# Softmax division moved behind the value product: a factor spread by DMA, one multiply of x on GpSimd, and shorter lags

## The chip, the cores and the metric

One core of a Trainium2 chip runs the whole program. The metric is the device time in microseconds (us) of one launch; lower is better. The engines are called PE (TensorE), PEld (its weight load), DVE (VectorE), ACT (ScalarE), POOL or Pool (GpSimd) and SP (the queue that issues the DMAs).

## What is computed

Attention over 16 heads of 768 tokens and 64 features, in which a query sees only the keys with the same 6-bit hash of sign bits, followed by two MLPs of 512, 2048 and 512 features over 1536 tokens:

```python
q_bits = (np.einsum('bhsd,dk->bhsk', q, proj) > 0)      # the same for k; a bucket is the 6 bits
mask = q_bucket[:, :, :, None] == k_bucket[:, :, None, :]
scores = np.where(mask, scale * np.matmul(q, k.transpose(0, 1, 3, 2)), -1000000000.0)
attn = np.exp(scores - np.max(scores, axis=-1, keepdims=True))
attn = attn / (np.sum(attn, axis=-1, keepdims=True) + 1e-09)
x = np.matmul(attn, v)                                  # heads side by side: (1536, 512)
x = gate_1(x @ w_in) @ w_out                            # gate_1: 0, (h + 1)^2 / 4 or h
return (lambda h: h - np.tanh(h))(x @ w_in2) @ w_out2
```

## The kernel before

All products are done in pairs of a rounded high part and a remainder ("hi" and "lo"), so nearly every operand is split by a rounding copy and a subtraction. The kernel has two stages. This case is about the first, the attention; the MLPs follow from about 260 us on and are PE's products one after the other.

**Pairs and steps.** The 16 heads are worked off as 8 pairs. A pair has 12 tiles of 128 queries by 768 keys (`PT_TILES`), tiles 0 to 5 of its first head (s = 0) and 6 to 11 of its second (s = 1). Each engine runs its own loop over n = 0 to 11 in `pair(p)`; I call one turn a step. In step n PE makes the scores of tile n (`scores`, 4 matmuls), then one third of a value product of an older tile (`weighted_values`, 4 matmuls), then the 6 transposes of another older tile (`transposes`). After steps 5 and 7 it also makes the bit products of the next pair (`bit_products`). Which older tile it is, is set by lags: the operation for tile o stands in step o + lag, and runs over into the next pair.

**A tile's way.** DVE takes the masked scores from PSUM and finds the row's least value (`clamp`), ACT takes the exponential and the row's sum (`exponent`), DVE inverts the sums of three tiles at a time (`invert`, a `tensor_scalar` called row_den here and a reciprocal), Pool multiplies the tile by the inverse (`normalise`, lag 3), PE transposes it (lag 5) into two PSUM banks e = 0 and 1, ACT rounds each bank (`parts_hi`), DVE subtracts (`parts_lo`), and only then is that bank free for the next tile's transposes. After three tiles PE has what it needs for the value product (lag 9, over three steps); ACT copies its lower half out (`lower_half`) and DVE adds it to the upper one (`fold`, lag 11) into x_pair. x_pair holds both heads: partitions 0 to 63 the first, 64 to 127 the second, with the queries along the free side. In step 9 ACT rounds the last pair's x_pair (`round_x`), and Pool subtracts (`split_x`).

**Pool and SP.** The order of every engine is written out by hand in `pair`. Between its `normalise` instructions Pool splits q, k and v of the coming heads (`split_q`, `split_k`, `split_v`): in steps 0 and 1 for the second head of this pair, in steps 6 and 7 for the first head of the next. ACT makes the rounded k for it (`round_k`). SP waits for the split, copies the rounded q and the bits into place (`copy_q_hi`, `copy_bits`) and then issues the next loads; PE's first scores of a head wait for those copies. The last pair is followed by a drain: the loops run once more for what lags, PE mixes in the first products of the MLP (`early_hidden`), and Pool splits the MLP's weights (`split_w`), the first two of them already in steps 5 and 7 of the last pair.

## Time and profile before

| | |
|---|---|
| three runs, median (range) | 784.14 us (783.81 to 784.57) |
| the profiled execution | 784.89 us, of it 783.0 us in the profile's span |
| PE busy, by the page | 757.5 us (97%) |
| DVE, ACT, POOL busy | 422.3 (54%), 356.3 (46%), 327.2 us (42%) |
| granted clock of PE | 0.995 over the span |

The shares are means over both stages. Up to about 245 us DVE, ACT and Pool are busy most of the time too; behind it PE alone is.

### The profile page before, as it was taken

To read this page: it belongs to the slowest core of one execution; us is meant where nothing else is said; L and a number is where in the kernel's file an instruction comes from. 1 tells how busy PE (TensorE), PEld (TensorE's weight loads), DVE (VectorE), ACT (ScalarE), POOL (GpSimd) and SP (SyncE) were. 2 spreads that over 40 slices of the span, in tenths; PEclk is the share of its full clock that TensorE was granted. 3 is DMA by queue.
4 is the path that set the end of the run, shared out by engine and by line. 5 is a ranking of instruction groups with operands and counts; after the bars stand their busy time and mean duration, and the time that the engine had idled before them with its cause. 6 is when DMAs were issued, how large, how long until landed. Compare 5 with 4: busy or idle time off the path is not lost.

```text
span 783.0 us, 11765 instructions
## 1 busy us (share of the span) xinstructions
PE 757.5 (97%) x3712; PEld 636.5 (81%) x3712; DVE 422.3 (54%) x757; ACT 356.3 (46%) x701; POOL 327.2 (42%) x267
## 2 busy tenths in 40 slices
PE   4999999999999999999999999999999999999998
PEld 2788888888888888878887888878888888888886
DVE  2899999999997565353334455551123221231213
ACT  2889889889887333343334333331122221221212
POOL 4789889889899995000000176770000000000000
PEclk8999999999999999999999999999999999999999
DMA  5533523523222333000000032220000000010001
GB/s 191 173 118 106 162 76 106 162 76 106 82 83 75 128 120 109 0 1 1 0 1 0 0 107 85 102 81 1 0 1 32 23 0 0 0 54 0 0 0 54
DMA packets 17864, 47.25 MB, mean 60 GB/s; under 512 B 2288, under 2 KB 4464, under 8 KB 17840
## 3 DMA queue, kind: packets, MB, share of 16 engines
q1 hardware_dynamic: 17840, 46.94, 18.7%
q8 instruction: 14, 0.23, 0.1%
q14 instruction: 10, 0.08, 0.0%
HBM read 38.87 MB, written 3.15 MB: 54 GB/s over the span
## 4 chain that ended last, share of the span: by engine, by line
PE 81%; POOL 5%; issue 5%; DVE 4%; ACT 3%; DMA 2%; SPq 1%; DVEq 0%; POOLq 0%; ACTq 0%
PE ps L498 33%; PE ps L575 30%; PE ps L475 5%; PE ps L489 5%; PE ps L461 2%; PE ps L464 2%; PE ps L432 2%; POOL probs L355 2%; POOL k_b L340 1%; ACT probs L620 1%; DMA k_raw<-kk 1%; DVE g_raw L814 1%; DVE row_den L744 1%; ACT g_hi L702 1%; POOL q_b L312 1%
## 5 line engine op out<-in xcount | busy, mean ns | idle before, releaser
L498 PE MATMUL ps<-x_hi,w 128*128 (+1 forms) x768 | 249.7, 390 | 0.0
L822 DVE TENSOR_TENSOR g_lo<-g_raw,g_hi 128x512 fp32r<-128x512 f32 x96 | 72.6, 756 | 261.5 <-ACT g_hi L702 261.5
L702 ACT ACTIVATE g_hi<-g_raw 128x512 fp32r<-128x512 f32 x96 | 60.7, 632 | 287.9 <-PE ps L575 262.7
L498 PEld LDWEIGHTS ps<-x_hi,w 128*128 128x128 f32 x768 | 144.1, 188 | 29.7
L498 PE MATMUL ps<-x_lo,w 128*128 (+1 forms) x384 | 149.4, 389 | 0.0
L575 PE MATMUL ps<-g_hi,w 128*128 128x512 f32 x384 | 125.2, 390 | 2.5 <-DVE g_lo L822 2.5
L575 PE MATMUL ps<-w,g_hi 128*128 128x512 f32 x384 | 118.2, 389 | 0.0
L312 POOL TENSOR_SCALAR w<-stage 128x1024 fp32r<-128x1024 f32 x32 | 39.0, 1217 | 159.1 <-PE ps L575 157.9
L752 DVE TENSOR_TENSOR p_lo<-ps,p_hi 128x384 fp32r<-128x384 f32 x192 | 97.9, 552 | 9.7 <-ACT p_hi L630 8.1
L355 POOL TENSOR_SCALAR probs<-probs,row_inv 128x768 f32<-128x768 f32 x96 | 86.9, 909 | 23.9 <-DVE row_inv L746 22.9
L630 ACT ACTIVATE p_hi<-ps 128x384 fp32r<-128x384 f32 x192 | 84.7, 489 | 25.0 <-PE ps L475 22.9
L736 DVE TENSOR_SCALAR_CACHE_REDUCE clamped<-ps 128x768 f32<-128x768 f32 x96 | 91.0, 949 | 6.0 <-PE ps L464 5.9
L620 ACT ACTIVATE probs<-clamped,row_min 128x768 f32<-128x768 f32 x96 | 90.2, 939 | 8.6 <-DVE clamped L736 8.6
L475 PE MATMUL ps<-ident,probs 128*128 128x128 f32 x576 | 82.3, 277 | 7.4 <-POOL probs L355 3.8
L575 PEld LDWEIGHTS ps<-g_hi,w 128*128 128x128 f32 x384 | 72.1, 188 | 19.1 <-DVE g_lo L822 4.1
L370 POOL TENSOR_TENSOR w<-stage,w 128x1024 fp32r<-128x1024 f32 x32 | 83.8, 2620 | 2.7
L575 PEld LDWEIGHTS ps<-w,g_hi 128*128 128x128 f32 x384 | 72.1, 188 | 14.9
L498 PEld LDWEIGHTS ps<-x_lo,w 128*128 128x128 f32 x384 | 72.1, 188 | 14.7
L475 PEld LDWEIGHTS ps<-ident,probs 128*128 128x128 f32 x576 | 65.6, 140 | 20.8 <-DVE p_lo L752 11.0
L575 PE MATMUL ps<-g_lo,w 128*128 128x512 f32 x192 | 74.7, 389 | 0.0
L575 PE MATMUL ps<-w,g_lo 128*128 128x512 f32 x192 | 74.7, 389 | 0.0
L814 DVE TENSOR_TENSOR g_raw<-g_mid,g_raw 128x512 f32<-128x512 f32 x48 | 52.3, 1089 | 33.5 <-ACT g_mid L696 33.5
(48 smaller groups left out, 902.6 us busy)
## 6 DMA issues: line engine op xcount, KB each, us to landing
stage<-weights SPq DMA_DIRECT2D x32, 512.0 KB, 3.3
qk_raw<-qk SPq DMA_DIRECT2D x16, 384.0 KB, 3.5
q_raw<-qq SPq DMA_DIRECT2D x16, 384.0 KB, 3.1
k_raw<-kk SPq DMA_DIRECT2D x16, 384.0 KB, 3.8
q_a<-q_b SPq DMA_DIRECT2D x16, 192.0 KB
v_raw<-v SPq DMA_DIRECT2D x16, 192.0 KB, 2.7
out<-stage SPq DMA_DIRECT2D x12, 256.0 KB, 2.1
q_b<-bits SPq DMA_DIRECT2D x16, 54.0 KB
```

What stands on the lines that cost most here:

```text
L355: pool.tensor_scalar(probs[:, o % QT, :], probs[:, o % QT, :], row_inv[:, o % QT:o % QT + 1], 1.0, ALU.mult, ALU.mult).then_inc(probs_read ...
L370: pool.tensor_tensor(w[:, slot, 1, :], stage[:, i, :], w[:, slot, 0, :].bitcast(F32), ALU.subtract).then_inc(w_ready, 1)
L475: last = nc.tensor.transpose(part_bank(o, e)[:, j * P:(j + 1) * P], probs[:, o % QT, kt * P:(kt + 1) * P], ident[:, :])
L498: last = nc.tensor.matmul(ps[:, f % H_BANKS, :], w[:, f, wp, k * P:(k + 1) * P], xs[:, k, bass.ds(t * TOK, TOK)], start=(k == 0 and wp == ...
L575: last = nc.tensor.matmul(ps[:, 4 + m, :], a, b, start=(f == 0 and i == 0), stop=(f == FC - 1 and i == 2))
L620: nc.scalar.activation(probs[:, n % QT, :], clamped[:, n % 2, :], ACT.Exp, bias=row_min[:, n % QT:n % QT + 1], scale=-1.0, accum_out=row_s ...
L630: nc.scalar.activation(p_hi[:, k % 2, HT * e:HT * (e + 1), i, :], part_bank(o, e).rearrange("p (j q) -> p j q", j=HT), ACT.Copy)\
L702: nc.scalar.activation(g_hi[:, slot, :], g_raw[:, slot, :], ACT.Copy).then_inc(g_hi_ready, 1)
L736: nc.vector.tensor_scalar(clamped[:, n % 2, :].rearrange("p (c n) -> p c n", c=2), score_bank(TURNS.index(n)), FLOOR, None, ALU.min, ALU.m ...
L752: nc.vector.tensor_tensor(p_lo[:, k % 2, HT * e:HT * (e + 1), i, :], part_bank(o, e).rearrange("p (j q) -> p j q", j=HT), p_hi[:, k % 2, H ...
L814: nc.vector.tensor_tensor(g_raw[:, slot, :], g_mid[:, slot, :], g_raw[:, slot, :], ALU.add)\
L822: nc.vector.tensor_tensor(g_lo[:, slot, :], g_raw[:, slot, :], g_hi[:, slot, :].bitcast(F32), ALU.subtract).then_inc(g_split, 1)
```

## The change

`normalise` is gone, and PE transposes the exponentials as they are, as soon as ACT has made them. The inverse of the row sums is made once for a head (6 tiles) instead of once for three tiles. SP stores it to memory (`store_inv`, 128 partitions of 6 numbers) and loads it back, so that every one of the head's 64 partitions of x_pair has all 768 factors beside its queries (`spread_inv`, into inv_wide). Pool then multiplies x_pair by it, in two halves of 384 queries (`scale_x`, steps 5 and 9 of the next pair), where the inverse is read with a step of 6 numbers. ACT's rounding and Pool's subtraction of x go in halves too. Pool makes the rounded k itself, which ACT did. The lags go from 5, 9 and 11 to 4, 8 and 10. ACT and DVE do the parts of a step ahead of the fold, and DVE inverts last. In the drain DVE scales the last pair's x.

```diff
@@ -54,10 +54,10 @@
-SCALE_LAG = 3
-TRANSPOSE_LAG = 5
-PV_LAG = 9
-FOLD_LAG = 11
+TRANSPOSE_LAG = 4
+PV_LAG = 8
+FOLD_LAG = 10
+SCALE_TURNS = [5, 9]
...
-            row_sum = sb("row_sum", [P, QT], F32, att)
-            row_den = sb("row_den", [P, QT], F32, att)
-            row_inv = sb("row_inv", [P, QT], F32, att)
+            row_sum = sb("row_sum", [P, 2, QT], F32, att)
+            row_den = sb("row_den", [P, 2, QT], F32, att)
+            row_inv = sb("row_inv", [P, 2, QT], F32, att)
+            inv_wide = sb("inv_wide", [P, S], F32, att)
+            x_tiles = x_pair[:, :].rearrange("p (o q) -> p o q", o=QT)
+            inv_tiles = inv_wide[:, :].rearrange("p (q o) -> p o q", o=QT)
...
+            def store_inv(p, s):
+
+                sp.wait_ge(inv_ready, 2 * p + s + 1)
+                sp.dma_start(factors[2 * p + s, :].rearrange("(q o) -> q o", o=QT), row_inv[:, s, :])\
+                    .then_inc(inv_stored[s], 16)
+
+            def spread_inv(p, s):
+
+                sp.wait_ge(inv_stored[s], 16 * (p + 1))
+                if s == 0:
+                    wait_from(sp, x_scaled, 2 * p)
+                sp.dma_start(inv_wide[s * D:(s + 1) * D, :], factors[bass.ds(2 * p + s, 1), :].broadcast_to([D, S]))\
+                    .then_inc(inv_spread, 16)
...
+                first = isinstance(p, int) and p == 0
                 sp.wait_ge(qk_split, 2 * p + 2)
                 copy_q_hi(1)
                 copy_bits(1)
+                if not first:
+                    store_inv(p - 1, 1)
+                if not last:
+                    load_qk(2 * p + 3, 1)
+                if not first:
+                    spread_inv(p - 1, 1)
                 if last:
                     return
-                load_qk(2 * p + 3, 1)
...
                 copy_q_hi(0)
                 copy_bits(0)
+                store_inv(p, 0)
                 if not before:
                     load_qk(2 * p + 4, 0)
+                spread_inv(p, 0)
                 sp.wait_ge(v_split, 2 * p + 2)
                 load_v(2 * p + 3, 1)
...
             load_w(0, 0)
             load_w(1, 1)
+            for s in range(2):
+                store_inv(PAIRS - 1, s)
+                spread_inv(PAIRS - 1, s)
...
             def split_k(p, s):
+                pool_round(k_a[:, s, :], k_raw[:, s, :]).then_inc(k_hi_ready, 1)
...
-            def normalise(p, o):
-
-                wait_alone(pool, inv_ready, 4 * p + o // HT + 1, pool_passed)
-                pool.tensor_scalar(probs[:, o % QT, :], probs[:, o % QT, :], row_inv[:, o % QT:o % QT + 1], 1.0,
-                                   ALU.mult, ALU.mult).then_inc(probs_ready, 1)
-
-            def split_x(p):
-                pool.wait_ge(x_hi_ready, p + 1)
-                pool.tensor_tensor(x_lo_flat[:, bass.ds(rows(p), S)], x_pair[:, :],
-                                   x_hi_flat[:, bass.ds(rows(p), S)].bitcast(F32), ALU.subtract)\
-                    .then_inc(x_ready, 1)
+            def scale_x(p, half):
+
+                cols = slice(half * HT, (half + 1) * HT)
+                wait_alone(pool, folded, 4 * p + 3 + half, pool_passed)
+                wait_alone(pool, inv_spread, 32 * (p + 1), pool_passed)
+                pool.tensor_tensor(x_tiles[:, cols, :], x_tiles[:, cols, :], inv_tiles[:, cols, :], ALU.mult)\
+                    .then_inc(x_scaled, 1)
+
+            def split_x(p, half):
+                pool.wait_ge(x_hi_ready, 2 * p + half + 1)
+                run = bass.ds(rows(p) + half * HALF, HALF)
+                pool.tensor_tensor(x_lo_flat[:, run], x_pair[:, half * HALF:(half + 1) * HALF],
+                                   x_hi_flat[:, run].bitcast(F32), ALU.subtract).then_inc(x_ready, 1)
...
-                    old = trailing(p, n, SCALE_LAG)
-                    if old and not (drain and n >= SCALE_LAG):
-                        normalise(*old)
+                    old = trailing(p, 0, 1)
                     if not drain:
+                        if old and n in SCALE_TURNS:
+                            scale_x(old[0], SCALE_TURNS.index(n))
...
+                        if old and n == 7:
+                            split_x(old[0], 0)
                         if n == 7 and not last:
                             split_k(p + 1, 0)
                         if n == 10 and not last:
                             scale_q(p + 1, 1)
+                        if old and n == 10:
+                            split_x(old[0], 1)
                         if n == 11:
                             split_v(p, 1)
-                        if last and n in (5, 7):
-                            split_w((n - 5) // 2)
-                    if n == 9 and not drain:
-                        old = trailing(p, 0, 1)
-                        if old:
-                            split_x(old[0])
+                        if last and n in (5, 8):
+                            split_w((n - 5) // 3)
...
             pair(PAIRS - 1)
-            pair(PAIRS, drain=True)
...
             def transposes(p, o):
-                pe.wait_ge(probs_ready, PT_TILES * p + o + 1)
+                pe.wait_ge(exp_done, PT_TILES * p + o + 1)
...
-            def round_k(p, s, tiles_before):
+            def round_k(p, s):
                 act.wait_ge(qk_loaded[s], 32 * (p + 1))
-                wait_from(act, scores_ready, tiles_before)
                 nc.scalar.activation(k_a[:, s, :], k_raw[:, s, :], ACT.Copy).then_inc(k_hi_ready, 1)
-            def round_x(p):
-                act.wait_ge(folded, 4 * (p + 1))
-                nc.scalar.activation(x_hi_flat[:, bass.ds(rows(p), S)], x_pair[:, :], ACT.Copy)\
-                    .then_inc(x_hi_ready, 1)
+            def round_x(p, half):
+                act.wait_ge(x_scaled, 2 * p + half + 1)
+                nc.scalar.activation(x_hi_flat[:, bass.ds(rows(p) + half * HALF, HALF)],
+                                     x_pair[:, half * HALF:(half + 1) * HALF], ACT.Copy).then_inc(x_hi_ready, 1)
...
-                act.wait_ge(folded, 4 * PAIRS - 1 + half)
+                act.wait_ge(x_last_scaled, half + 1)
...
-                    if n == 9 and not drain:
-                        old = trailing(p, 0, 1)
-                        if old:
-                            round_x(old[0])
-                    if n in (6, 9) and drain:
-                        round_last_x((n - 6) // HT)
-                    old = trailing(p, n, FOLD_LAG)
-                    if n % HT == HT - 1 and old and not (drain and n >= FOLD_LAG):
-                        lower_half(old[0], old[1] // HT)
                     old = trailing(p, n, TRANSPOSE_LAG)
                     if old and not (drain and n >= TRANSPOSE_LAG):
                         parts_hi(*old)
+                    old = trailing(p, n, FOLD_LAG)
+                    if old and old[1] % HT == 0 and not (drain and n >= FOLD_LAG):
+                        lower_half(old[0], old[1] // HT)
+                    old = trailing(p, 0, 1)
+                    if old and n - 1 in SCALE_TURNS and not drain:
+                        round_x(old[0], SCALE_TURNS.index(n - 1))
+                    if drain and n in (FOLD_LAG - 5, FOLD_LAG - 2):
+                        round_last_x((n - FOLD_LAG + 5) // HT)
                     if not drain:
-                        if n == 0:
-                            round_k(p, 1, PT_TILES * p)
-                        if n == 6 and not (isinstance(p, int) and p == PAIRS - 1):
-                            round_k(p + 1, 0, PT_TILES * p + QT)
                         exponent(p, n)
...
-            def invert(p, k):
-
-                cols = slice((k % 2) * HT, (k % 2 + 1) * HT)
-                dve.wait_ge(exp_done, PT_TILES * p + HT * (k + 1))
-                nc.vector.tensor_scalar(row_den[:, cols], row_sum[:, cols], 1e-9, None, ALU.add).then_inc(den_ready, 1)
-                dve.wait_ge(den_ready, 4 * p + k + 1)
-                nc.vector.reciprocal(row_inv[:, cols], row_den[:, cols]).then_inc(inv_ready, 1)
+            def invert(p, s):
+
+                dve.wait_ge(exp_done, PT_TILES * p + QT * (s + 1))
+                nc.vector.tensor_scalar(row_den[:, s, :], row_sum[:, s, :], 1e-9, None, ALU.add).then_inc(den_ready, 1)
+                dve.wait_ge(den_ready, 2 * p + s + 1)
+                wait_from(dve, inv_stored[s], 16 * p)
+                nc.vector.reciprocal(row_inv[:, s, :], row_den[:, s, :]).then_inc(inv_ready, 1)
...
-                if k == 0:
-                    wait_from(dve, x_ready, p)
+                if k < 2:
+                    wait_from(dve, x_ready, 2 * p - 1 + k)
                 nc.vector.tensor_tensor(x_pair[r:r + D, c:c + HALF], ps[0:D, PV0 + k % 2, 0:HALF], low[:, k % 2, :], ALU.add)\
                     .then_inc(folded, 1)
+            def scale_last_x(half):
+
+                cols = slice(half * HT, (half + 1) * HT)
+                dve.wait_ge(folded, 4 * PAIRS - 1 + half)
+                dve.wait_ge(inv_spread, 32 * PAIRS)
+                nc.vector.tensor_tensor(x_tiles[:, cols, :], x_tiles[:, cols, :], inv_tiles[:, cols, :], ALU.mult)\
+                    .then_inc(x_last_scaled, 1)
...
-                    if n in (6, 9) and drain:
-                        split_last_x((n - 6) // HT)
                     if not drain:
                         clamp(p, n)
-                    old = trailing(p, n, FOLD_LAG)
-                    if n % HT == HT - 1 and old and not (drain and n >= FOLD_LAG):
-                        fold(old[0], old[1] // HT)
-                    old = trailing(p, n, HT)
-                    if n % HT == 0 and old and not (drain and n >= HT):
-                        invert(old[0], old[1] // HT)
                     old = trailing(p, n, TRANSPOSE_LAG)
                     if old and not (drain and n >= TRANSPOSE_LAG):
                         parts_lo(*old)
+                    old = trailing(p, n, FOLD_LAG)
+                    if old and old[1] % HT == 0 and not (drain and n >= FOLD_LAG):
+                        fold(old[0], old[1] // HT)
+                    if drain and n in (FOLD_LAG - 6, FOLD_LAG - 3):
+                        scale_last_x((n - FOLD_LAG + 6) // HT)
+                    if drain and n in (FOLD_LAG - 5, FOLD_LAG - 2):
+                        split_last_x((n - FOLD_LAG + 5) // HT)
+                    old = trailing(p, n, QT)
+                    if n % QT == 0 and old and not (drain and n > 0):
+                        invert(old[0], old[1] // QT)
                     if not drain and n in BITS_AFTER and not last:
                         threshold(p + 1, BITS_AFTER.index(n))
```

On Pool, in the middle pairs (pairs 1 to 6), steps 6 to 9. Before:

```order
L77 ISA [waits scores_ready]
L312 TENSOR_SCALAR q_b<-q_raw 128x768 [waits q_scaled]
L327 TENSOR_TENSOR q_a<-q_raw,q_b 128x768 [waits q_hi_ready]
L355 TENSOR_SCALAR probs<-probs,row_inv 128x768 [waits inv_ready]
L340 TENSOR_TENSOR k_b<-k_raw,k_a 128x768 [waits k_hi_ready]
L355 TENSOR_SCALAR probs<-probs,row_inv 128x768 [waits inv_ready]
L77 REGISTER_ALU
L355 TENSOR_SCALAR probs<-probs,row_inv 128x768 [waits inv_ready]
L360 ISA [waits x_hi_ready]
L360 TENSOR_TENSOR x_lo<-x_pair,x_hi 128x768
```

And with the change, from step 5 on (L390 is `scale_x`, L396 `split_x`, L344 the rounding copy):

```order
L390 TENSOR_TENSOR x_pair<-x_pair,inv_wide 128x384 [waits inv_spread]
L77 REGISTER_ALU
L77 ISA [waits scores_ready]
L344 TENSOR_SCALAR q_b<-q_raw 128x768 [waits q_scaled]
L359 TENSOR_TENSOR q_a<-q_raw,q_b 128x768 [waits q_hi_ready]
L394 ISA
L396 ISA [waits x_hi_ready]
L396 TENSOR_TENSOR x_lo<-x_pair,x_hi 128x384
L344 TENSOR_SCALAR k_a<-k_raw 128x768
L373 TENSOR_TENSOR k_b<-k_raw,k_a 128x768 [waits k_hi_ready]
```

The three `normalise` instructions left the stretch; the first half of x is now multiplied ahead of the split of the next head, and its remainder is made inside it, between q and k.

On SP, at the top of a middle pair. Before:

```order
L238 DMA q_a<-q_b 64x768 [waits qk_split]
L244 DMA q_b<-bits 18x768
L244 DMA k_b<-bits 18x768
L227 ISA
L227 DMA q_raw<-qq 128x768
L227 DMA k_raw<-kk 128x768
L271 REGISTER_ALU
L230 ISA [waits v_split]
L230 DMA v_raw<-v 128x384
```

And with the change:

```order
L244 DMA q_a<-q_b 64x768 [waits qk_split]
L250 DMA q_b<-bits 18x768
L250 DMA k_b<-bits 18x768
L255 ISA
L256 ISA [waits inv_ready]
L256 DMA factors<-row_inv 128x6
L233 ISA
L233 DMA q_raw<-qq 128x768
L233 DMA k_raw<-kk 128x768
L261 REGISTER_ALU
L264 DMA inv_wide<-factors 64x768 [waits inv_stored1]
```

The store of the last head's inverse stands behind the three copies, the loads behind it, and the spread behind the store's landing.

## Rows read from the trace of the kernel before

**Rows 1.** Busy time by stretch: pair 0, pairs 1 to 6 (five periods), the rest.

```profile
core 0: us, PE busy (x) PEld busy (x) DVE busy (x) ACT busy (x) POOL busy (x), PEclk, DMA share, GB/s
16.50:39.80 23.30, 21.60 (x111) 17.71 (x111) 19.03 (x45) 16.89 (x37) 17.33 (x18) 0.89 0.64 185
52.80:198.90 146.10, 142.21 (x882) 126.42 (x881) 139.61 (x311) 127.21 (x276) 129.99 (x126) 1.00 0.37 115
199.00:243.80 44.80, 42.10 (x265) 37.80 (x263) 43.00 (x97) 38.86 (x86) 40.90 (x38) 1.00 0.27 85
```

**Rows 2.** Timeline of PE: the bit products behind step 5 of pairs 1 and 6.

```profile
52.77 0.49 PE L432 MATMUL ps<-qk_raw,mask_s 128*72 128x384 f32 x1
...
198.93 0.81 PE L432 MATMUL ps<-qk_raw,mask_s 128*72 128x384 f32 x2
```

**Rows 3.** The chain that ended last, pair 5: start us, us, what.

```profile
169.86 1.29 PE ps L432 x4
171.15 0.35 PE ps L461 x2
171.50 0.36 PE ps L464 x2
171.86 0.70 PE ps L489 x4
172.57 0.66 PE ps L475 x6
```

**Rows 4.** Who waited for whom, 52.8 to 198.9 us: total, times, longest.

```profile
PEld ps L475 <- DVE p_lo L752: 9.8, 25, 0.7
...
PE ps L475 <- POOL probs L355: 2.1, 5, 0.4
```

**Rows 5.** Timeline of DVE in pair 5: start, duration, instruction.

```profile
158.17 0.99 DVE L744 TENSOR_SCALAR row_den<-row_sum 128x3 f32<-128x3 f32 x1
...
162.05 0.95 DVE L736 TENSOR_SCALAR_CACHE_REDUCE clamped<-ps 128x768 f32<-128x768 f32 x1
...
162.93 0.55 DVE L763 TENSOR_TENSOR x_pair<-ps,low 64x384 f32<-64x384 f32 x1
163.43 1.02 DVE L752 TENSOR_TENSOR p_lo<-ps,p_hi 128x384 fp32r<-128x384 f32 x2
164.37 0.95 DVE L736 TENSOR_SCALAR_CACHE_REDUCE clamped<-ps 128x768 f32<-128x768 f32 x1
...
165.24 0.69 DVE L744 TENSOR_SCALAR row_den<-row_sum 128x3 f32<-128x3 f32 x1
...
172.93 0.16 DVE L744 TENSOR_SCALAR row_den<-row_sum 128x3 f32<-128x3 f32 x1
```

**Rows 6.** Timeline of POOL in the same pair.

```profile
158.12 1.01 POOL L349 TENSOR_TENSOR v_s<-v_raw,v_s 128x384 fp32r<-128x384 f32 x1
...
160.45 0.83 POOL L312 TENSOR_SCALAR q_b<-q_raw 128x768 fp32r<-128x768 f32 x1
...
164.07 1.84 POOL L340 TENSOR_TENSOR k_b<-k_raw,k_a 128x768 fp32r<-128x768 f32 x1
```

**Rows 7.** Timeline of ACT in the same pair.

```profile
163.67 0.94 ACT L620 ACTIVATE probs<-clamped,row_min 128x768 f32<-128x768 f32 x1
...
165.57 0.94 ACT L620 ACTIVATE probs<-clamped,row_min 128x768 f32<-128x768 f32 x1
```

**Rows 8.** DMA issues of the whole run: KB each, median us to landing.

```profile
k_raw<-kk SPq DMA_DIRECT2D x16, 384.0 KB, 3.8
...
v_raw<-v SPq DMA_DIRECT2D x16, 192.0 KB, 2.7
out<-stage SPq DMA_DIRECT2D x12, 256.0 KB, 2.1
```

**Rows 9.** Timeline of SP's queue in the same pair.

```profile
165.94 0.53 SPq L238 DMA_DIRECT2D q_a<-q_b  x1
...
167.32 0.70 SPq L244 DMA_DIRECT2D k_b<-bits  x1
```

**Rows 10.** Costliest groups of the whole run: busy, mean ns.

```profile
L370 POOL TENSOR_TENSOR w<-stage,w 128x1024 fp32r<-128x1024 f32 x32 | 83.8, 2620 | 2.7
```

21 lines of the change are left out of this document (13 added, 8 removed).

## The prediction

> **What bounds the kernel now.** I read the busy times by stretch first [rows 1]: from 52.8 to 198.9 us PE is busy 97% of the time and DVE 96%, so neither has room, and the attention is where the two wait for each other. The two bit products that bound this stretch stand at the same place of pairs 1 and 6 [rows 2], so it holds five pairs, and a pair takes (198.93 - 52.77) / 5 = 29.2 us.
>
> Next, what would a pair take if PE never waited? The chain, where it runs along PE [rows 3], gives a step: scores 0.35 + 0.36, a third of a value product 0.70, transposes 0.66, together 2.07 us; and 1.29 us for a bit product, of which a pair has two. 12 x 2.07 + 2 x 1.29 = 27.4 us. So a pair has 1.8 us of stalls. The waits say whose they are [rows 4]: the weight loads of the transposes wait 9.8 us in five pairs, 2.0 a pair, for DVE's p_lo, which frees their PSUM bank, and the transposes 2.1 us, 0.4 a pair, for Pool's `normalise` (these overlap a little). The larger part is thus a late DVE, not a late Pool.
>
> Why is DVE late? Its own step [rows 5]: clamp to the next instruction 162.93 - 162.05 = 0.88, two p_lo 164.37 - 163.43 = 0.94, together 1.82 us in a step of 2.07. There is 0.25 us of room a step. A fold takes 163.43 - 162.93 = 0.50 of it. And row_den, an instruction on 3 numbers a partition, takes 0.16 us once, but 0.99 and 0.69 us at other times. The longer two end at 159.16 and 165.93; Pool's instructions that were running [rows 6] end at 158.12 + 1.01 = 159.13 and 164.07 + 1.84 = 165.91. So row_den waits until Pool's instruction in progress is over. That is 0.8 and 0.5 us lost on the path from p_lo to the transposes.
>
> **What the change does to a pair.** Pool loses 12 `normalise` a pair, and with them the wait of 0.4 us a pair on PE disappears. The path from the exponential to the transposes has nothing but ACT in it now. That is sure.
>
> DVE: 4 row_den and 4 reciprocals become 2 and 2. But they stand in steps 0 and 6, just where Pool runs four instructions on end for a head: q_b 0.83, q_a and k_b 1.84 [rows 6], and the rounded k as long as q_b. A row_den that falls there at random waits on average (0.83^2 + 1.84^2) / (2 x 2.67) = 0.76 us, at least 0, at most 1.84. In sum 2 x 0.76 against some 1.3 for the two of before: DVE gains only what two short pairs of instructions cost, under 0.7 us a pair. The place matters too: behind p_lo, the delay meets the next clamp and the next p_lo. As p_lo may come about 0.6 us late before PE feels it (2.07 - 1.82 and the slack between its end and the transposes, an estimate), a row_den that costs 0.16 + 0.2 for the reciprocal + 0.76 = 1.1 us stalls PE by 0.5 in step 0. In step 6 the same is hidden by the bit product behind step 7, 1.29 us of PE against one short DVE instruction. The folds of steps 1 and 4 add perhaps 0.1.
>
> ACT: exponential to exponential it takes 165.57 - 163.67 = 1.90 us [rows 7] of 2.07. The two rounded k of a pair leave it; x comes in two halves, of which the one in step 10 stands behind a `lower_half` and should cost PE about 0.1. So 1.8 us of stalls become 0.6 (0.5 + 0.1, the rest hidden); a pair takes 28.0 us. **Per pair: -1.2 us.**
>
> **The new round trip.** The half of step 5 needs the factor, which needs Pool, SP, two DMAs one behind the other. I count from PE's first scores of a pair, t = 0. Pool reaches the split at about t = 2.4: step 10 of the pair before starts at 10 x 2.07 + 2 x 1.29 = 23.3, its transposes 1.4 later, ACT's two parts, lower half and half of x end at about 27.0 (an estimate from one ACT step of 1.9), and Pool's remainder and v follow, 1.0 + 1.6, to 29.6, which is 2.2 to 2.4 of the next pair. It takes 5.5 us to 7.9. SP's copies take from 165.94 to 167.32 + 0.70 [rows 9], 2.1 us, to 10.0. The store lands like the smallest HBM store, 2.1 us [rows 8], at 12.1; the spread like v, of the same 192 KB, 2.7, at 14.9, with the loads of q and k ahead of it at most 1 us later. A DMA that writes 24 bytes a partition is not in the trace: its landing lies between nothing and the longest row, 3.8, and I take the store's. The multiply has the size of v's remainder, 1.0 us [rows 6]: done at 15.9. ACT wants it at about 16.5 (step 6, behind its parts). Then Pool goes on: q 2.75, the remainder of x 1.0, k 2.75 to 22.4, copies to 24.5, landed some 1.7 later (an estimate from the first head) at 26.3; PE wants it at 27.4. So the trip fits, with about 1 us to spare, and costs nothing while it does.
>
> The multiply reads inv_wide in steps of 24 bytes, which no row of before does. Below it is bounded by 0.5 (half of v's remainder), above by the 1.84 of an instruction of twice the size. I take 1.0, as its sizes are those of v's remainder. By the Trainium skill (GPSIMD Engine Reference, section Performance pitfalls for Q7 kernels), a read of SBUF by steps of over 8 bytes costs about half as much again on GpSimd; no trace here shows it. By that rule the multiply would take 1.5 instead of 1.0 us, and the sum would stay where it is, with half of the spare time gone.
>
> For the row_den the Trainium skill (SBUF — State Buffer, section Who interferes with whom) names an exclusive lock of the port pair that VectorE and GpSimd share, for `tensor_scalar` among others, held for a whole instruction. The trace agrees with it [rows 5, 6]. The rule goes further than the rows: it lets a VectorE instruction with both inputs in SBUF wait in the same way, which concerns the last pair's multiply only.
>
> **The ends.** Pair 0: a shorter lag puts one group of transposes and one third of a value product, 1.36 us [rows 3], into the start, where PE has 23.3 - 21.6 = 1.7 us idle [rows 1], and takes it from the drain, where PE is full. I take -0.8, between 0 and -1.7. The stretch from 199.0 to 243.8 is 44.8 / 28 = 1.6 pairs: -1.9. In the last pair Pool splits two weights of 2.62 us [rows 10] and a rounding each between the two multiplies; its second multiply is then ready about 1 to 2 us after ACT asks for it in step 10, with no bit products in that pair to hide it: +1.0. In the drain SP loads the third weight only behind the last spread, and DVE has one more multiply, of 1 us and a possible 2.6 of Pool's instruction, ahead of the first gate of the MLP: +0.4, between 0 and +3. The MLPs themselves are untouched.
>
> **Sum:** 5 x -1.2 = -6.0, -1.9, -0.8, +1.0, +0.4 = -7.3 us. The profiled execution took 784.89, 0.75 above the median of the three runs. 784.9 - 7.3 = 777.6, and 0.75 less on the scale of the median: 776.8.
>
> **Rivals.**
> 1. *Forecast*, stalls fall to 0.4 to 1.0 a pair: 773 to 781, chance 0.47.
> 2. *All stalls go.* If row_den finds Pool between instructions, or PE feels none of it: 27.4 a pair, -1.8 x 6.6 = -11.9, -0.8 in the start: 772 with the ends' losses, 769 without them and with 1.7 gained in the start. For it speaks that PE then waits for nothing that the change left; against it, that DVE would still be busy some 27 of 27.4 us. Chance 0.18.
> 3. *The gain is eaten* by row_dens at their upper bound: 2 x 1.84 puts DVE at 29 us a pair, the same as now. With the ends' +1.4 and -0.8, 781 to 785, chance 0.15.
> 4. *Slower: a late factor.* Where: Pool's multiply of step 5, with q, k and the copies of the next head queued behind it and ACT's exponentials behind the rounding of step 6. The spare time is about 1 us and the stalls of before 1.8, so from 2.9 us of lateness on it decides against the change. Both DMAs at 3.8 instead of 2.1 + 2.7 are +2.8, the multiply at 1.84 +0.8: 3.6 late, a pair of 27.4 + 2.6 = 30.0, +0.8 x 6.6 = +5.3, and with the ends about 790. A middle value of these is 785 to 788. Chance 0.16.
> 5. *The slow stride alone*: the multiply lies between v's remainder, 1.0, and the 1.84 of twice the size [rows 6], so about 0.5 us more for each half, and with the loads ahead of the spread ACT gets x 0.5 to 0.9 us late in step 6. Stall up to 0.5 a pair, 6.6 x 0.5 = 3.3: 780. Chance 0.04, beside what 1 holds of it. The GPSIMD Engine Reference of the Trainium skill, cited above, is what speaks for it.
>
> **Numbers.** The likeliest is 776.8. Its own range is 773 to 781; the range for 8 in 10 takes in rivals 2 and 3 and the start of 4: 769 to 787. A measurement of this kernel tells about 0.2%, 1.6 us, from no change. Faster by more than that (below 782.6): 1, 2, 5 and half of 3, 0.76. Within it: the rest of 3 and a little of 4, 0.09. Slower: 0.15.
>
> **What would show it.** In the profile after: a pair of about 28.0 us between bit products; no wait of the transposes for Pool, and that for DVE's p_lo down from 2.0 to about 0.7 a pair; two row_dens a pair of 0.2 to 2 us, each ending with an instruction of Pool; the multiply at about 1.0 us and ACT's rounding of x without a wait for it, except once in the last pair. Wrong would be: PE's scores waiting for the copied bits (rival 4), ACT waiting for x in every pair, or the multiply at 1.5 and more. The step I trust least is the round trip's spare microsecond.

## The result and the profile after

The changed kernel took 793.18 us (median of 4 runs, 790.28 to 794.71), the kernel before 783.97 us beside it (783.63 to 784.57): a ratio of 1.0108, 95% interval 1.0093 to 1.0123. It is slower by 9 us, where 776.8 had been forecast and 787 was the end of the range. The profiled execution took 794.71 us, the slowest of the four, with a span of 792.5 us, 9.5 more than before.

Busy time by stretch, after the change; the stretches are those of [rows 1], shifted to the same places of the program, with one for the drain:

```profile
core 0: us, PE busy (x) PEld busy (x) DVE busy (x) ACT busy (x) POOL busy (x), PEclk, DMA share, GB/s
16.50:39.80 23.30, 21.51 (x109) 18.15 (x110) 19.13 (x38) 15.37 (x34) 13.13 (x13) 0.85 0.66 187
55.30:202.60 147.30, 143.25 (x883) 126.31 (x882) 138.93 (x291) 123.56 (x272) 97.69 (x90) 1.00 0.45 123
202.60:248.70 46.10, 41.80 (x266) 38.06 (x263) 42.84 (x89) 38.11 (x86) 30.41 (x27) 1.00 0.24 70
```

Five pairs took 147.3 us instead of 146.2. Pool was rid of a quarter of its work there, 130.0 to 97.7 us. DVE was rid of 0.7 us in five pairs and no more. The timeline of PE has the bit products that answer to [rows 2]:

```profile
55.28 1.13 PE L466 MATMUL ps<-qk_raw,mask_s 128*72 128x384 f32 x3
...
202.56 1.13 PE L466 MATMUL ps<-qk_raw,mask_s 128*72 128x384 f32 x3
```

From such marks the whole run can be cut up: the bit products of pair 0, those of pairs 1 and 6, PE's first product of the MLP with x (hidden), its first product of g (project), the end. The same cuts serve for every kernel below. The differences are of the marks themselves, before rounding.

| us | before | after | difference | predicted |
|---|---|---|---|---|
| start to the bits of pair 0 | 25.2 | 26.2 | +1.0 | 0 |
| bits of pair 0 to bits of pair 1 | 27.5 | 29.1 | +1.5 | -0.8 |
| a pair, mean of five | 29.23 | 29.46 | +0.23 (x5: +1.1) | -1.2 (x5: -6.0) |
| bits of pair 6 to first hidden | 47.4 | 49.1 | +1.7 | -0.9 |
| first hidden to first project | 20.8 | 25.0 | +4.2 | +0.4 |
| first project to the end | 515.8 | 515.8 | 0 | 0 |

The first row is the start's own scatter (24.1 to 28.2 us over all kernels here, with no order by their edits). It goes largely with the clock that PE was granted from 5 to 28 us: 0.85 in the kernel before and 0.78 after, 0.85 in experiment 9, which has the shortest start (24.1), and 0.70 in experiment 7 (27.8), though 12, the longest, had 0.78. The waits of the changed kernel from 55.3 to 202.5 us, which answer to [rows 4]:

```profile
PEld ps L509 <- DVE p_lo L780: 9.9, 30, 1.1
...
PE ps L509 <- DVE p_lo L780: 4.0, 5, 0.8
...
ACT x_hi L679 <- POOL x_pair L390: 2.2, 4, 0.7
```

No transpose waits for Pool any more: that step came true. But PE waits as long for p_lo as before, at fewer and longer stops. One is in the timelines of DVE, POOL and PE of a pair:

```profile
162.70 1.32 DVE L771 TENSOR_SCALAR row_den<-row_sum 128x6 f32<-128x6 f32 x1
164.15 0.19 DVE L774 RECIPROCAL row_inv<-row_den 128x6 f32<-128x6 f32 x1
164.35 0.96 DVE L764 TENSOR_SCALAR_CACHE_REDUCE clamped<-ps 128x768 f32<-128x768 f32 x1
...
165.24 1.02 DVE L780 TENSOR_TENSOR p_lo<-ps,p_hi 128x384 fp32r<-128x384 f32 x2
```

```profile
162.16 1.84 POOL L359 TENSOR_TENSOR q_a<-q_raw,q_b 128x768 fp32r<-128x768 f32 x1
```

```profile
165.84 1.01 PE L509 MATMUL ps<-ident,probs 128*128 128x128 f32 x6 [0.80 <-DVE p_lo L780]
```

row_den ends at 164.02, with Pool's q_a at 164.00; six numbers a partition took 1.32 us. Clamp and p_lo follow late, and PE stops for 0.80 us. The ten row_dens of the stretch took 0.95 us in the mean; the twenty of before, on half as many numbers, 0.50. Half the instructions, each twice as long: DVE won nothing. The mean hides a fixed pattern: the row_den of step 0 took 1.32 or 1.33 us in each of the five pairs, always to the end of q_a, and the one of step 6 took 0.17 to 0.78.

The round trip, in the timelines of SP's queue, POOL and ACT in pair 5 (PE's first scores of the pair at 158.97):

```profile
166.74 0.53 SPq L244 DMA_DIRECT2D q_a<-q_b  x1
167.31 0.79 SPq L250 DMA_DIRECT2D q_b<-bits  x1
168.15 0.73 SPq L250 DMA_DIRECT2D k_b<-bits  x1
169.19 0.37 SPq L256 DMA_DIRECT2D factors<-row_inv  x1
169.76 0.35 SPq L233 DMA_DIRECT2D q_raw<-qq  x1
170.20 0.38 SPq L233 DMA_DIRECT2D k_raw<-kk  x1
171.84 0.56 SPq L264 DMA_DIRECT2D inv_wide<-factors  x1
```

```profile
176.35 1.21 POOL L390 TENSOR_TENSOR x_pair<-x_pair,inv_wide 128x384 f32<-128x384 f32 x1 [7.25 <-DMA inv_wide<-factors]
```

```profile
177.69 0.53 ACT L679 ACTIVATE x_hi<-x_pair 128x384 f32 x1 [0.53 <-POOL x_pair L390]
```

The inverse was ready at 164.34 and its store was issued at 169.19: 4.9 us it stood behind SP's wait for the split. Then store 2.65 us (169.19 to 171.84, where the spread leaves), spread 4.5 (to the multiply's start at 176.35), multiply 1.21. How the first two share the time differs from pair to pair: at the same place of the pair before, the store landed in 1.4 us and the spread in 5.4, here in 2.6 and 4.3. Their sum does not: from the store's issue to the spread's landing it took 6.9 to 7.1 us at this place in each of the five pairs. The page's table of DMA issues has the medians of the whole run; its first row answers to that of [rows 8]:

```profile
k_raw<-kk SPq DMA_DIRECT2D x16, 384.0 KB, 5.2
...
inv_wide<-factors SPq DMA_DIRECT2D x16, 192.0 KB, 4.6
...
factors<-row_inv SPq DMA_DIRECT2D x16, 3.0 KB, 1.7
```

So the store is a short transfer as a rule, and the spread, behind the 768 KB of q and k, the long one.

The last pair has the longest stop. Pool splits a weight there, DVE's row_den waits for it, and PE's scores wait for the clamp behind (timelines of POOL, DVE, PE):

```profile
235.49 2.38 POOL L405 TENSOR_TENSOR w<-stage,w 128x1024 fp32r<-128x1024 f32 x1
```

```profile
236.17 1.72 DVE L771 TENSOR_SCALAR row_den<-row_sum 128x6 f32<-128x6 f32 x1
```

```profile
239.05 0.61 PE L495 MATMUL ps<-k_a,q_a 128*128 128x384 f32 x2 [2.00 <-DVE clamped L764]
```

In the drain SP issued the third and fourth weight only behind the last spread, at 253.87, where the kernel before had issued them at 233.74 and 239.41. Pool got its weight at 258.73, and PE stopped twice (timelines of SP's queue, POOL, PE; then busy time by stretch):

```profile
253.04 0.47 SPq L264 DMA_DIRECT2D inv_wide<-factors  x1
253.87 0.90 SPq L320 DMA_DIRECT2D stage<-weights  x2
```

```profile
258.73 1.67 POOL L344 TENSOR_SCALAR w<-stage 128x1024 fp32r<-128x1024 f32 x1 [9.06 <-DMA stage<-weights]
```

```profile
267.42 0.50 PE L532 MATMUL ps<-x_hi,w 128*128 128x512 f32 x1 [1.25 <-POOL w L405]
...
272.23 0.50 PE L532 MATMUL ps<-x_hi,w 128*128 128x512 f32 x1 [1.78 <-POOL w L405]
```

```profile
272.20:276.70 4.50, 4.47 (x13) 3.55 (x14) 3.04 (x4) 1.75 (x3) 4.42 (x3) 0.62 0.31 117
272.70:276.00 3.30, 3.30 (x10) 2.56 (x9) 1.83 (x4) 1.75 (x3) 3.22 (x2) 0.50 0.42 159
```

Behind the second stop PE ran at half its clock from 272.7 to 276.0 us. At full clock it starts three of these products every 0.69 us, there every 1.28, so this alone is some 1.5 us of the drain's 4.2 (an estimate from the rows at the end of this document), and it belongs to this execution: no other kernel below had such a fall between hidden and project, and of the eleven others that issue the third weight as late, none needed more than 22.3 us there.

### The profile page after: what moved, and what is told of

The parts are those of the page before. It is cut to its first block, busy times and chain, and to the rows that moved or that the text cites. A ratio compares the mean times of both kernels' runs of the same rounds, so it can differ in the third digit from the quotient of the medians.

```text
span 792.5 us, 11668 instructions
## 1 busy us (share of the span) xinstructions
PE 760.3 (96%) x3712; PEld 638.3 (81%) x3712; DVE 428.5 (54%) x727; ACT 350.5 (44%) x693; POOL 273.4 (34%) x207
## 2 busy tenths in 40 slices
DMA packets 21447, 50.44 MB, mean 64 GB/s; under 512 B 4848, under 2 KB 7024, under 8 KB 21424
## 4 chain that ended last, share of the span: by engine, by line
PE 84%; DVE 5%; issue 3%; ACT 3%; DMA 2%; POOL 1%; SPq 0%; DVEq 0%; ACTq 0%; POOLq 0%
PE ps L532 32%; PE ps L609 30%; PE ps L509 7%; PE ps L523 6%; PE ps L495 4%; PE ps L498 4%; PE ps L466 2%; DVE p_lo L780 1%; DMA stage<-weights 1%; DVE row_den L771 1%; DVE clamped L764 1%; DMA k_raw<-kk 1%; DVE g_raw L852 1%; ACT g_hi L730 1%; POOL w L405 1%
## 5 line engine op out<-in xcount | busy, mean ns | idle before, releaser
L780 DVE TENSOR_TENSOR p_lo<-ps,p_hi 128x384 fp32r<-128x384 f32 x192 | 97.7, 550 | 12.9 <-ACT p_hi L664 12.7
L344 POOL TENSOR_SCALAR w<-stage 128x1024 fp32r<-128x1024 f32 x32 | 39.9, 1246 | 166.9 <-PE ps L609 155.1
L664 ACT ACTIVATE p_hi<-ps 128x384 fp32r<-128x384 f32 x192 | 84.8, 488 | 28.2 <-PE ps L509 27.3
L609 PEld LDWEIGHTS ps<-w,g_hi 128*128 128x128 f32 x384 | 72.1, 188 | 14.9
L852 DVE TENSOR_TENSOR g_raw<-g_mid,g_raw 128x512 f32<-128x512 f32 x48 | 54.2, 1129 | 33.5 <-ACT g_mid L724 33.5
L495 PE MATMUL ps<-k_a,q_a 128*128 128x384 f32 x192 | 60.5, 397 | 10.1 <-DMA k_b<-bits 6.2
```

Source lines behind the costliest of these rows:

```text
L495: nc.tensor.matmul(score_bank(turn)[:, c, :], q_a[:, s, q], k_a[:, s, c * HALF:(c + 1) * HALF], start=True, stop=False)
L609: last = nc.tensor.matmul(ps[:, 4 + m, :], a, b, start=(f == 0 and i == 0), stop=(f == FC - 1 and i == 2))
L664: nc.scalar.activation(p_hi[:, k % 2, HT * e:HT * (e + 1), i, :], part_bank(o, e).rearrange("p (j q) -> p j q", j=HT), ACT.Copy)\
L780: nc.vector.tensor_tensor(p_lo[:, k % 2, HT * e:HT * (e + 1), i, :], part_bank(o, e).rearrange("p (j q) -> p j q", j=HT), p_hi[:, k % 2, H ...
L852: nc.vector.tensor_tensor(g_raw[:, slot, :], g_mid[:, slot, :], g_raw[:, slot, :], ALU.add)\
```

## The experiments

Times are medians; the ratio is to the kernel before, run on the same chip in the same jobs (783.97 to 784.86 us), with its 95% interval. The cuts are those of the table above, each from one profiled execution. Two kernels with the same code in a cut tell how far one execution can be trusted there: pair 0 took 29.1 us in the changed kernel and 27.9 in 2, which differs from it only behind the last pair, but the mean of five pairs 29.46 and 29.42.

| kernel | us | ratio | pair 0 | a pair | pair 6 to hidden | hidden to project |
|---|---|---|---|---|---|---|
| before | 783.97 | | 27.5 | 29.23 | 47.4 | 20.8 |
| after | 793.18 | 1.0108 [1.0093, 1.0123] | 29.1 | 29.46 | 49.1 | 25.0 |
| 1 no row_den | 786.01 | 1.0013 [1.0004, 1.0023] | 26.7 | 29.22 | 48.0 | 21.4 |
| 2 weights first | 790.25 | 1.0072 [1.0055, 1.0088] | 27.9 | 29.42 | 50.2 | 20.4 |
| 3 both of these | 785.44 | 1.0017 [1.0002, 1.0032] | 26.7 | 29.16 | 47.4 | 20.3 |
| 4 before, no row_den | 780.11 | 0.9939 [0.9923, 0.9956] | 27.3 | 28.60 | 46.7 | 20.8 |
| 5 lags 5, 9, 11 | 783.47 | 0.9987 [0.9978, 0.9997] | 27.2 | 28.90 | 46.9 | 21.3 |
| 6 store first | 787.46 | 1.0040 [1.0020, 1.0059] | 28.4 | 29.22 | 47.7 | 21.8 |
| 7 store first, no row_den | 779.35 | 0.9926 [0.9910, 0.9943] | 26.7 | 28.02 | 46.2 | 22.2 |
| 8 all three edits | 777.42 | 0.9904 [0.9887, 0.9920] | 26.7 | 28.02 | 46.2 | 20.8 |
| 9 all three, lags 5, 9, 11 | 776.53 | 0.9902 [0.9885, 0.9919] | 26.6 | 28.14 | 46.0 | 20.8 |
| 10 no row_den, lags 5, 9, 11 | 778.50 | 0.9915 [0.9898, 0.9931] | 26.2 | 28.28 | 46.0 | 21.3 |
| 11 lags 4, 9, 11 | 835.85 | 1.0646 [1.0615, 1.0677] | 31.4 | 35.95 | 59.9 | 22.3 |
| 12 before, lags 4, 8, 10 | 805.45 | 1.0264 [1.0246, 1.0281] | 31.1 | 31.70 | 50.7 | 19.4 |
| 13 lags 4, 8, 11 | 785.36 | 1.0012 [1.0000, 1.0025] | 27.7 | 28.94 | 46.9 | 22.1 |
| 14 lags 5, 8, 10 | 803.45 | 1.0237 [1.0220, 1.0254] | 30.4 | 31.51 | 49.9 | 21.7 |
| 15 x_hi in step 11 | 799.99 | 1.0193 [1.0176, 1.0210] | 28.0 | 31.04 | 50.0 | 21.9 |
| 16 the same, lags 5, 9, 11 | 796.94 | 1.0150 [1.0127, 1.0173] | 27.7 | 30.71 | 51.5 | 21.4 |
| 17 x_hi in step 9 | 788.60 | 1.0056 [1.0040, 1.0073] | 28.2 | 29.30 | 47.4 | 21.4 |
| 18 all three, x_hi in step 9 | 775.26 | 0.9890 [0.9872, 0.9908] | 26.7 | 27.76 | 45.4 | 20.4 |

From the first project on every one of them took 515.8 to 516.0 us: the MLPs are untouched.

**1. Without row_den.** The sum of exponentials holds one exponential of 1, so 1e-9 vanishes in it.

```diff
-                nc.vector.tensor_scalar(row_den[:, s, :], row_sum[:, s, :], 1e-9, None, ALU.add).then_inc(den_ready, 1)
-                dve.wait_ge(den_ready, 2 * p + s + 1)
...
-                nc.vector.reciprocal(row_inv[:, s, :], row_den[:, s, :]).then_inc(inv_ready, 1)
+                nc.vector.reciprocal(row_inv[:, s, :], row_sum[:, s, :]).then_inc(inv_ready, 1)
```

> The changed kernel without row_den: the sum of a row is at least 1, so the added 1e-9 falls away in fp32, and the reciprocal reads the sums themselves. Everything else as in the changed kernel. Theory A (row_den, which waits for Pool's instruction in progress, is what keeps a pair at 29.5 us): the 0.95 us that it takes on average twice a pair go, a pair falls to 27.8 us or less, the total by 8 pairs x 1.6 to about 780. Rival B (the new order of ACT and DVE and the shorter lags keep the pair long): a pair stays above 29 us, the total within 2 us of the changed kernel, about 791.

7.2 us came back, between theory A and rival B. By the cuts it was 2.4 in pair 0, 1.1 from pair 6 to the MLP, 3.6 in the drain (of which some 1.5 are the clock of the one profiled execution, as above), but only 0.24 a pair. The stall had moved. In the timeline of ACT the exponentials now stand behind x_hi:

```profile
175.04 0.52 ACT L679 ACTIVATE x_hi<-x_pair 128x384 f32 x1 [1.63 <-POOL x_pair L390]
```

and the waits of five pairs have grown where those for p_lo shrank:

```profile
ACT x_hi L679 <- POOL x_pair L390: 7.3, 4, 2.4
PEld ps L509 <- DVE p_lo L778: 4.5, 18, 1.0
```

**2 and 3. Third and fourth weight loaded ahead of the last stores and spreads; the same without row_den.**

```diff
             load_w(1, 1)
+            for i in range(2):
+                sp.wait_ge(w_ready, i + 1)
+                load_w(2 + i, i)
             for s in range(2):
                 store_inv(PAIRS - 1, s)
                 spread_inv(PAIRS - 1, s)
-            with sp.Fori(1, FC) as c2:
+            with sp.Fori(2, FC) as c2:
```

> The changed kernel, with the loads of the third and fourth weight issued on SP ahead of the last pair's stores and spreads of the factor, as they were before the change. Theory A (the drain loses its 4 us because those loads stand behind the factor's round trip): the wait of PE for Pool's weights goes, the first projection of the MLP moves from 276.7 to about 271, the total falls by 4 to 6 us to about 788. Rival B (the drain is late for the multiply of x on DVE ahead of the first gate): the total falls by less than 1.5 us.

> Both edits, no row_den and the weights' loads first. If the two losses are independent, the total is the changed kernel less the sum of both gains: 793 - 12 - 5 = about 776, faster than the kernel before. If one hides the other, it is above that by what it hides.

With the weights first, hidden to project is 20.4 us instead of 25.0, as before the change, and the two stops are gone; 1.1 us went back ahead of the MLP. In the times it gave 2.9 us, less than the 4 to 6 of theory A, and the runs of the two touch (789.62 to 790.37 against 790.28 to 794.71). In 3 the 776 of two independent losses was missed by 9 us: beside experiment 1 the edit gave nothing that the times can tell (786.01 and 785.44): without row_den the drain took only 21.4 us as it was.

**4. The kernel before without row_den.**

```diff
-                nc.vector.tensor_scalar(row_den[:, cols], row_sum[:, cols], 1e-9, None, ALU.add).then_inc(den_ready, 1)
-                dve.wait_ge(den_ready, 4 * p + k + 1)
```

> The kernel before, without row_den, all else as it was. Theory A (row_den costs both kernels): the long row_dens of 0.99 and 0.69 us in a pair go, and the inverse reaches Pool earlier, so the total falls by about 1 us a pair, to about 776. Rival B (Pool's multiply of the tiles keeps PE waiting anyway): less than 2 us.

780.11 us, 0.63 a pair less, where theory A had 776. So row_den cost the kernel before about 4 us and the changed one 7: doing it half as often in longer pieces did not make it cheaper.

**5. The old lags in the changed kernel.** `TRANSPOSE_LAG`, `PV_LAG`, `FOLD_LAG` at 5, 9, 11.

> The changed kernel with the lags of before, 5, 9 and 11, all else as changed. Theory A (the shorter lags cost nothing in a pair and only move 1.4 us of PE's work from the drain to the start): a pair stays at 29.5 us, the start is up to 1.4 us shorter, the drain as much longer, the total within 1.5 us of the changed kernel, 791.7 to 794.7. Rival B (the shorter lags make the stalls): a pair falls below 29 us and the total by 3 us or more.

9.7 us came back, the rival's side by far, and against the prediction, in which the shorter lags were a gain.

**6, 7 and 8. The store ahead of the wait for the split.** 6 alone, 7 without row_den, 8 with the weights first as well.

```diff
+                if not first:
+                    store_inv(p - 1, 1)
                 sp.wait_ge(qk_split, 2 * p + 2)
                 copy_q_hi(1)
                 copy_bits(1)
                 if not first:
-                    store_inv(p - 1, 1)
-                if not last:
-                    load_qk(2 * p + 3, 1)
-                if not first:
                     spread_inv(p - 1, 1)
+                if not last:
+                    load_qk(2 * p + 3, 1)
```

> The changed kernel with SP's order at the top of a pair turned: the store of the factor first, ahead of the wait for the split, and the spread ahead of the loads of q and k. row_den stays. Theory A (with row_den in place the round trip just fits, as ACT waits only 0.5 us for x in step 6): Pool's multiply of step 5 comes 3 to 4 us earlier, PE gains less than 0.3 us a pair, the total is 791 to 793. Rival B (the trip already holds the pair up): the total falls by 4 us or more.

> The same order on SP, and no row_den. Theory A (without row_den the late factor is what keeps a pair at 29.2 us: ACT waited up to 2.4 us for x in step 6): that wait goes, a pair falls to 27.8 us, the total to about 786 - 8 x 1.3 = 776. Rival B (something else, such as p_lo waiting for p_hi, holds it): a pair stays above 28.8 us, the total above 783.

> All three edits: no row_den, the store first, the weights' loads first. If the theory of three losses holds (row_den, the late factor, the late weights), a pair takes 27.8 us, the first projection of the MLP comes at about 259 us instead of 276.7, and the total is 773 to 776, below the kernel before and below the kernel before without row_den (780.1).

6 alone gave 5.7 us, rival B's side in the total (4 or more) and theory A's in a pair (less than 0.3): the rest stood outside the five pairs. 7 and 8 missed their 776 and 773 to 776 by 3.4 and 1.4 us.

This is the reading of the pairs. Without row_den alone a pair takes 29.22 us, with the store first alone 29.22, with both 28.02. Each of the two costs hides the other: taken one at a time they are worth 0.24 us a pair, together 1.44. In 8 the timelines of SP's queue and POOL show the trip with the store made early and the spread ahead of the loads:

```profile
155.45 0.36 SPq L256 DMA_DIRECT2D factors<-row_inv  x1
...
161.44 0.56 SPq L264 DMA_DIRECT2D inv_wide<-factors  x1
162.21 0.41 SPq L233 DMA_DIRECT2D q_raw<-qq  x1
```

```profile
164.77 1.20 POOL L393 TENSOR_TENSOR x_pair<-x_pair,inv_wide 128x384 f32<-128x384 f32 x1 [3.30 <-DMA inv_wide<-factors]
```

The multiply starts 3.3 us after the spread's issue, not 4.5, with nothing ahead of it, and there is no wait of ACT for x left in five pairs. The edit did two things, the store ahead of the wait and the spread ahead of the loads; they were not run apart.

**9 and 10. The old lags with all three edits, and with row_den dropped alone.**

> The changed kernel without row_den, with the store of a head's inverse ahead of the wait for the split, with the third and fourth weight loaded before the last round trip, and with lags of 5, 9 and 11. Theory A (the lags cost time only through where VectorE's row_den meets Pool's long instructions): without row_den the lags are worth nothing in a pair, the period stays at 28.0 us, and only the half tile more of lag in the last pair and the drain moves the time, by up to 1 us either way: 776.5 to 778.5 us. Rival B (the longer lag gives ScalarE and VectorE room in each pair whatever row_den does): the period falls by the 0.5 us that the lags gave with row_den in place (29.46 to 28.9), the time by 3 us or more, to 774 us or less.

> The changed kernel without row_den and with lags of 5, 9 and 11, nothing else. Without row_den at 4, 8 and 10 it took 786.0 us, with row_den at 5, 9 and 11 it took 783.5. Theory A (both remove the same waits): the time lies within 1 us of the better one less the round trip's cost, 782 to 785 us. Rival B (two separate costs that add): 786.0 - 9.7, or some 776 to 778 us. In the waits ScalarE's wait for x on Pool, 7.3 us in all without row_den, tells how much of the rest is the round trip.

With all three edits the lags are worth less than a microsecond, and in a pair nothing (28.14 against 28.02), as theory A had it. But in 10 they gave 7.5 us without any row_den: theory A's ground, that they act through row_den, has fallen, and rival B came within 0.5 us of the time. That they act where the trip is tight is a reading that fits both, and the table of places below.

**11 and 12. Transposes alone at 4; the lags of 4, 8 and 10 in the kernel before.**

> The changed kernel with the transposes 4 tiles behind, and the products with v and the folds put back to 9 and 11. Theory A (what the old lags gave comes of the transposes' distance from the exponentials: with 5 the chain exp, transpose, rounding, p_lo has a tile more of slack against VectorE's row_den): little changes from the changed kernel, 791 to 794 us. Rival B (it comes of the fold and the products with v, which at 10 put the last fold of a head and the inverse closer to Pool's split and take a tile more from pair 0): most of the 9.7 us comes, 783 to 786 us.

> The kernel before with lags of 4, 8 and 10, and nothing else of the change. In it Pool still multiplies each tile of probabilities one turn ahead of the transpose (2.1 us of waits of the transposes for Pool in five pairs with a lag of 5). Theory A (the shorter lag by itself costs: a chain of one tile less): 787 to 793 us, with TensorE's waits for p_lo and for the scaled tiles grown by 3 us or more. Rival B (the short lag costs only together with the changed order of ScalarE and VectorE and the long row_den of the changed kernel): within 2 us of the kernel before, 783 to 786 us.

Both lie outside what either theory gave, for reasons of their own, which the waits name (over a stretch of some 147 us, which holds four pairs of 11 and not quite five of 12). In 11 a group's products with v end one step behind the transposes that want its buffer:

```profile
ACT p_hi L664 <- PE ps L523: 38.6, 16, 4.0
```

In 12 Pool's `normalise` has one step instead of two ahead of the transposes:

```profile
POOL probs L355 <- DVE row_inv L746: 26.1, 19, 2.9
...
PE ps L475 <- POOL probs L355: 10.9, 21, 1.3
```

So it is the change that makes the short lags possible, and 11 can't be read as a test of the fold.

**13 and 14. One lag put back at a time: the fold's to 11; the transposes' to 5.**

> The changed kernel with only the fold (and ScalarE's copy low ahead of it) put back from 10 tiles to 11; transposes stay at 4, products with v at 8. The old lags together gave 9.7 us (793.2 to 783.5). Theory A (it is where the fold falls: at 10 the copy low, 0.49 us, stands in step 10 of ScalarE beside x_hi, 0.51 us, and the fold, 0.55 us, stands in the step right behind VectorE's row_den; at 11 neither meets): most of it comes, 783 to 786 us. Rival B (it is the transposes' lag, the slack between exponential and transpose): it stays at 791 to 794 us.

> The changed kernel with only the transposes put back from 4 tiles to 5; products with v stay at 8, folds at 10. Theory A (the place of the fold): 791 to 794 us, no gain. Rival B (the slack between exponential and transpose, the chain p_hi, p_lo): 783 to 786 us. With the fold run beside it, the two tell whether the 9.7 us are one cause's or a sum.

The fold's lag alone brings 7.8 of the 9.7 us, 0.52 in a pair. 14 is lost to a wait that neither theory had: with transposes at 5 the products with v, at 8, come too soon for p_lo (15.2 us of waits in five pairs), so it says nothing of the rest.

**15 and 16. x_hi one step later, at lags 4, 8, 10 and at 5, 9, 11.** ACT's copy `low` and x_hi share step 10 at a fold lag of 10, and no step at 11; 15 parts them, 16 joins them.

```diff
-SCALE_TURNS = [5, 9]
+SCALE_TURNS = [5, 10]
...
-                        if old and n == 10:
+                        if old and n == 11:
                             split_x(old[0], 1)
```

> The changed kernel with the multiply of a head's second half in Pool's step 10 in place of 9, ScalarE's rounding x_hi in step 11 in place of 10, and Pool's x_lo in step 11; lags stay at 4, 8 and 10. ScalarE's step 10 then holds only one of low (0.49 us) and x_hi (0.51 us). Theory A1 (that meeting is what the lag of 10 costs): 5 of the 7 pairs' worth of some 0.5 us and the last pair come back, 788 to 791 us. Rival B (the meeting is harmless, as ScalarE has room): 792 to 794 us.

> The converse: lags of 5, 9 and 11 (783.5 us) with the same shift of the multiply to step 10 and of x_hi to step 11, where ScalarE's low of a fold at 11 stands. Theory A1 (low and x_hi in one step cost): 786 to 789 us. Rival B: 783 to 784.5 us.

Both got slower by much more than either theory said, 6.8 and 13.5 us. A little of it may be the clock: in the profiled executions of 14, 15 and 16 PE was once granted 0.50 for 3.3 us and more in the attention (in 15 at 187.8 to 191.1), in that of 11 three times. What 15 and 16 moved besides is Pool: it stands in its queue at x_lo until x_hi is done, with v and the next head's split behind it. The waits of five pairs in 15:

```profile
POOL x_lo L396 <- ACT x_hi L679: 24.3, 6, 6.2
...
ACT x_hi L679 <- POOL x_pair L390: 13.3, 4, 3.9
```

The first row alone is no sign of a loss: 6, which is faster, has 24.1 us there. It is one when ACT's wait for x grows with it, 2.2 us in the changed kernel and 13.3 here; in 6 there is none.

So there is a ring: second x_hi, x_lo, split, the copies, store, spread, multiply, and the first x_hi of the next pair, on which the exponentials wait. Whatever delays the second x_hi delays all of it, where the store waits for the split.

**17 and 18. x_hi one step earlier**, `SCALE_TURNS = [5, 8]`, alone and with the three edits of 8.

> The changed kernel with the multiply of a head's second half in Pool's step 8 in place of 9 and ScalarE's rounding x_hi in step 9 in place of 10; lags stay at 4, 8 and 10, x_lo stays in Pool's step 10. On Pool nothing changes places except beside the weight splits of the last pair; on ScalarE x_hi stands a step ahead of low. Moved to step 11 it cost 6.8 us, since Pool's x_lo, and with it the next head's split and the trip, came later too (Pool waited up to 6.2 us for x_hi). Theory C (the last x_hi sets when Pool gets to x_lo and the next split, and that starts the trip): Pool's wait for x_hi in five pairs falls from 13.6 us to 3 to 7, x_hi's own wait for the multiply grows little, and the time falls to 785 to 789 us. Rival D (the fold at 10 costs by its place behind row_den on VectorE, not by x_hi): 791 to 794 us.

> The version with all three edits (no row_den, store first, weights first; 777.4 us, pair period 28.0) with x_hi at step 9 and the multiply at step 8. There the trip has its slack back already (no wait of ScalarE for x on Pool), so theory C gives little in a pair: 776 to 778 us. Rival D gives the same; above 779 us would say that x_hi at 9 has come to wait for the multiply.

17 gained 4.6 us, in theory C's range, with Pool's wait for x_hi at 9.5 us (3 to 7 were expected). But only 0.15 us of it came in each pair, which is rival D's answer; the rest came in pair 0, the last pair and the drain, where one profiled execution tells least. 18 is the fastest of all, 775.26 us, 1.1% faster than the kernel before and just below the 776 to 778 expected; its runs (774.97 to 777.31) overlap those of 8 (776.69 to 777.64), so the step's own gain there, 2 us, is likely but not sure.

**Where x stands in a pair.** The timelines of one pair of each kernel, start in us from the bit products behind its step 5 (173.08 in the changed kernel), with the row_den ahead of them:

| kernel | second x_hi | split | multiply | first x_hi | row_den, us long | a pair |
|---|---|---|---|---|---|---|
| after | -15.1 | -11.8 | +3.3 | +4.6 | 1.32 | 29.46 |
| 1 no row_den | -13.9 | -10.6 | +4.4 | +5.7 | none | 29.22 |
| 6 store first | -15.1 | -11.8 | +0.4 | +4.0 | 1.31 | 29.22 |
| 7 both | -13.9 | -10.6 | +0.5 | +4.0 | none | 28.02 |
| 10 no row_den, old lags | -14.4 | -11.1 | +3.8 | +5.2 | none | 28.28 |
| 13 fold at 11 | -14.9 | -11.7 | +3.5 | +4.8 | 0.88 | 28.94 |
| 15 x_hi in step 11 | -12.4 | -9.1 | +6.7 | +8.0 | 0.55 | 31.04 |
| 17 x_hi in step 9 | -17.8 | -14.6 | +1.1 | +4.0 | 1.62 | 29.30 |

The last column is the mean of five pairs. The first x_hi stands at +4.0 wherever x is there in time. Rows 6 and 17 have it in time and a row_den of 1.3 to 1.6 us: 29.2 to 29.3 a pair. Row 1 has no row_den and x 1.7 us late: 29.2. Row 7 has neither: 28.0. Row 10 tells what the old lags do without row_den: `low`, 0.49 us, is no longer ahead of the second x_hi, which stands 0.5 us earlier, and so do split, multiply and first x_hi in the pair shown; in the mean of the five the first x_hi stands 0.86 us earlier, and a pair is 0.94 us shorter. Row 13 tells what the fold's lag does with it: x stands where it stood, but row_den is 0.44 us shorter, and a pair 0.52. Its end is set by Pool's q_a as before; DVE comes to it later.

## Why the prediction was wrong

**The removed wait.** Right. No transpose waits for Pool, in any run with the change.

**The step that failed: "So 1.8 us of stalls become 0.6 ...; a pair takes 28.0 us."** Measured 29.46. A pair of 28.0 exists: it is experiments 7 and 8, in which neither row_den nor the late store is left. The prediction had put row_den at 0.5 us of a pair and the late store at nothing. Measured by taking one away where the other is gone, each costs 1.2 us a pair (6 against 7, and 1 against 7: 29.22 and 28.02), and together 1.44, so that undoing one alone showed nothing. It is also luck that 28.0 is the number forecast: 0.5 of its 0.6 us of stalls were to be row_den's, and 7 has 0.6 without any.

- *row_den.* Its bound was right (nine of the ten end with an instruction of Pool, 0.17 to 1.33 us in five pairs). The mean of 0.95 us is close to the forecast 0.16 + 0.76, but not for its reason, an arrival at random: the one that matters for step 0 took 1.32 every time, 1.5 with the reciprocal where the sum had 1.1. What failed was that and its effect: "stalls PE by 0.5 in step 0" was 0.80 in the stop shown above, and a row_den took 1.7 us once each in pair 0 (at 30.23) and in the last pair, where Pool's weight split is longer still and PE stopped for 2.00 us. Those two places had been costed without it: pair 0 as -0.8, which is what it gives without row_den (26.7 against 27.5; 26.2 to 26.7 in all kernels with the change and no row_den), the last pair as +1.0 for another reason (a late multiply).
- *The trip.* "So the trip fits, with about 1 us to spare": from the split's end to the store's issue it was right (10.2 us after the pair's first scores, forecast 10.0), but store and spread took 2.65 + 4.5 = 7.2 us where the sum had 2.1 + 2.7 = 4.8. The rows it was read from were another kind: the store was taken from writes to `out`, the spread from loads of v. The store was not what was mis-sized (median 1.7 us, 2.65 in this pair); the spread was. It is slower than a load of v even with nothing just ahead of it (3.3 us in experiment 8 against 2.7), and behind q and k it took 4.2 to 5.6, where the prediction had named "at most 1 us" for them and left it out of the sum. Together they ran over by the spare microsecond and 1.4 us more; where row_den no longer made ACT late, ACT waited 1.63 us for x (experiment 1). This is rival 4's mechanism, in its place, but below the 2.9 us from which it was to decide. It decided nothing by itself; with row_den it took the whole gain.
- *The shorter lags.* Costed as a gain in pair 0 alone and as "perhaps 0.1" for the folds. Of all single edits, putting the old ones back gives most, 9.7 us, all of the loss. Shown: most of it is the fold's lag (13); it exists without row_den (10), and is gone once x is in time (9 against 8). How, the table of places tells: a fold lag of 10 puts `low` ahead of the second x_hi in step 10, which the prediction had seen and costed at "about 0.1" for PE, without following it round the ring to the next pair's first x_hi; and it lets DVE reach row_den earlier under Pool's q_a. The first is supported by 15 and 16 only in sign, the second by the positions of one pair in each kernel: no kernel moved `low` or the fold without the other. What the lag costs in the last pair and the drain is open.

**The ends.** The drain was costed at +0.4 between 0 and +3, and took +4.2. The cause had been named, the third weight behind the last spread; what was missed is that Pool needs 4 us for a weight once it lands. Experiment 2 shows that the late weights cost something: 20.4 us, and 2.9 us in the time, though 1 against 3 gives only 0.6 and 7 against 8 gives 1.9. The 4.2 overstates it: some 1.5 of it is the stretch at a granted clock of 0.50 in the one profiled execution. In the eleven other kernels with weights as late, and no such stretch, the drain took 21.3 to 22.3 us, 0.5 to 1.5 over the kernel before and within the forecast range. What makes the last 1.2 us of the 25.0 is open; one part is in the timelines: Pool's rounding of a weight took 1.67 and 1.70 us (at 258.73 and 263.03) beside DVE's two multiplies of x (258.56 and 262.80), and 1.05 elsewhere. The prediction had it the other way round, DVE's multiply waiting up to 2.6 us for Pool; it took 0.91 and 1.00.

**The multiply.** 1.0 us was taken, 1.21 measured, while v's remainder of the same sizes is still 1.0. By the Trainium skill (GPSIMD Engine Reference, section Performance pitfalls for Q7 kernels) it would have been 1.5; the trace shows a fifth more, not half. No run changed the stride alone.

**Rivals.** 2 did not happen. 3, "the gain is eaten by row_dens at their upper bound", had the sign of what happened in the pairs but not the way: the mean row_den was 0.95 us, half its bound. The costs of 1, 3 and 4 were weighed one by one; what happened was three moderate ones that meet in a ring. Rival 2's own terms give 772.8 and 770.5 us, not 772 and 769; nothing hangs on it.

The version with all three edits took 777.42 us, against a forecast of 776.8. That is another kernel, in which row_den, the late store and the late weights are gone, and the agreement speaks for the terms of the ends and of pair 0 rather than for the forecast of this one.

## What to carry to other kernels

A spare microsecond on a round trip has to be costed by transfers of the same kind in the same company, above all by what is queued ahead of them. When two waits can each hold the same engine, undoing one shows little; undo both before either is called harmless. Where the order of two engines is fixed, a wait of one for the other's instruction comes at the same place in every pair, and is better costed there than as a random arrival. And an engine that runs ahead and then stands at one instruction in its queue (Pool at x_lo) passes any delay there to everything behind it, so the step of that instruction matters more than its length.

## What the runs showed of the hardware

- A `tensor_scalar` of 128x6 on DVE took 0.16 us alone and 1.72 behind Pool's 2.38 us weight split, ending with it. The Trainium skill (SBUF — State Buffer, section Who interferes with whom) names such a lock, held for a whole instruction, and the trace agrees. A reciprocal of the same size took 0.19 us right behind it (at 237.93) while Pool's x_lo ran (237.83, 0.99 us).
- A store of 24 bytes a partition, 3 KB in all, took 1.7 us to its landing in the median of 16 (1.4 to 3.0), not much less than 256 KB of `out` at 2.1 [rows 8]. A spread of 3 KB over 64 partitions, 192 KB written, took 3.1 to 3.4 us with nothing just ahead (experiment 8, the second head's) and 4.2 to 5.6 behind the loads of q and k. The packets under 512 B went from 2,288 to 4,848, and q's and k's loads landed 1.1 and 1.4 us later than before. Whether the small packets or the spreads' bytes do that was not separated.
- After two stops of 1.25 and 1.78 us the granted TensorE clock was 0.50 from 272.7 to 276.0 us, the lower of its two levels of 1.2 and 2.4 GHz (0.62 is the mean over 4.5 us); the same products ran at 1.00 before the change. Two stops did not always do it: in experiment 7 they were 0.44 and 1.67 us at the same place, and the clock stayed at 1.00. In PE's timeline two products took 0.62 us at the one level and 1.06 at the other:

```profile
268.69 0.62 PE L532 MATMUL ps<-x_hi,w 128*128 128x512 f32 x2
...
269.38 0.62 PE L532 MATMUL ps<-x_hi,w 128*128 128x512 f32 x2
...
272.92 1.06 PE L532 MATMUL ps<-x_hi,w 128*128 128x512 f32 x2
...
274.20 1.06 PE L532 MATMUL ps<-x_hi,w 128*128 128x512 f32 x2
```
